# Routing and scatter moved into the delta rule of a one-core delta-rule and mixture-of-experts kernel

## What is computed

```python
# delta rule, k_n = k / (|k| + 1e-6), per batch and head
for t in range(S):
    y[t] = q[t] @ state
    state = state + beta[t] * outer(k_n[t], v[t] - k_n[t] @ state)
# experts: x is y as (3072, 384)
logits = x @ w_gate
e_idx = argmax(logits); gate_w = softmax(logits)[e_idx]
eom = 1 / (1 + exp(-(x @ w_output_gate)))
out[t] = gate_w * eom[t, e] * (relu(x[t] @ w1[e]) @ w2[e])      # e = e_idx[t]
# last layer
return maximum(maximum(out @ m1, out @ m2), out @ m3) @ w_out
```

## Time and profile before

| | before |
|---|---|
| runs, us | 1153.38, 1154.95, 1155.44 |
| median, us | 1154.95 |
| the profiled execution, us | 1154.56 |
| its span, us | 1152.8 |
| busy: PE, PEld, DVE, ACT, POOL, us | 1012.1, 887.3, 482.1, 366.7, 324.4 |
| mean granted clock of TensorE | 0.963 |
| stores of expert blocks (y_sorted<-y_sb) | 28 |
| memory read and written | 61.82 MB, 22.81 MB |

### The profile page before, as it was taken

The page is one execution under the profiler, slowest core; times in us unless marked ns, Lnnn a source line. Parts: engine busy times, 40 slices in busy tenths (PEclk is TensorE's granted clock), DMA queues, the critical chain, the costliest instruction groups (busy, mean ns, idle before and its releaser), DMA issues. The chain is left out here.

```text
span 1152.8 us, 30762 instructions
## 1 busy us (share of the span) xinstructions
PE 1012.1 (88%) x13236; PEld 887.3 (77%) x13236; DVE 482.1 (42%) x922; ACT 366.7 (32%) x731; POOL 324.4 (28%) x226
## 2 busy tenths in 40 slices
PE   1789999999998999810899999999599999999999
PEld 1678878888887888710799999999578888888888
DVE  3455555555555554360344344344242314242321
ACT  0255545555554555410222222222121212122211
POOL 2232333233422421046545255453420101000000
PEclk9999999999999999955899999999889999999999
DMA  8712121220212100016324344432211000100000
GB/s 267 269 54 63 28 60 40 62 63 26 63 40 62 41 20 19 2 42 232 136 81 155 122 151 151 150 124 82 89 49 35 28 34 20 34 20 28 10 19 28
DMA packets 59394, 86.37 MB, mean 75 GB/s; under 512 B 29200, under 2 KB 54288, under 8 KB 56720
## 3 DMA queue, kind: packets, MB, share of 16 engines
q1 hardware_dynamic: 53616, 48.46, 13.1%
q0 software_dynamic: 5664, 36.18, 9.2%
HBM read 61.82 MB, written 22.81 MB: 73 GB/s over the span
## 5 line engine op out<-in xcount | busy, mean ns | idle before, releaser
L1029 PE MATMUL hb<-early,last_h 128*128 128x512 f32 x648 | 203.8, 396 | 4.7 <-ACT o_sb L1143 3.5
L1029 PEld LDWEIGHTS hb<-early,last_h 128*128 128x128 f32 x648 | 120.5, 189 | 30.8 <-ACT o_sb L1143 2.7
L1029 PE MATMUL hb<-early,last_l 128*128 128x512 f32 x324 | 126.9, 392 | 0.0
L480 DVE TENSOR_TENSOR p<-bank,cf 128x512 f16<-128x512 f32 x96 | 66.0, 688 | 45.1 <-PE bank L283 44.8
L283 PEld LDWEIGHTS bank<-t,n_hi 64*64 64x64 f16 x2688 | 66.2, 111 | 21.1 <-issue 5.7
L1167 DVE TENSOR_TENSOR m<-hb,m 128x512 f32<-128x512 f32 x36 | 24.9, 691 | 131.4 <-PE hb L1029 131.4
L283 PE MATMUL bank<-t,n_hi 64*64 64x64 f16 x2688 | 71.6, 195 | 4.6 <-issue 3.9
L1029 PE MATMUL ob<-wo_h,early 128*128 128x384 f32 x288 | 74.2, 335 | 0.0
L1029 PEld LDWEIGHTS hb<-early,last_l 128*128 128x128 f32 x324 | 61.3, 189 | 13.2
L951 POOL TENSOR_TENSOR late<-w_raw,late 128x3072 fp32r<-128x3072 f32 x8 | 54.4, 6801 | 56.3 <-DVE late L923 56.0
L585 POOL COPY x_all<-y_tile 128x384 f32<-128x384 f32 x24 | 12.1, 503 | 205.3 <-ACT y_tile L451 205.3
(11 more groups left out here) (155 smaller groups left out, 2191.4 us busy)
## 6 DMA issues: line engine op xcount, KB each, us to landing
w_raw<-w POOLq DMA_DIRECT2D x14, 1536.0 KB, 7.6
kq_t<-qh SPq DMA_DIRECT2D x24, 256.0 KB, 3.3
x_sorted<-zeros SPq DMA_DIRECT2D x32, 192.0 KB, 1.9
x_in<-x_sorted SPq DMA_DIRECT2D x29, 192.0 KB, 2.4
y_sorted<-y_sb SPq DMA_DIRECT2D x28, 192.0 KB, 1.9
k_raw<-kt_in SPq DMA_DIRECT2D x24, 192.0 KB, 3.5
k_own<-kh SPq DMA_DIRECT2D x24, 192.0 KB, 3.3
v_in<-vh SPq DMA_DIRECT2D x24, 192.0 KB, 3.3
```

The lines of the kernel that those rows point to most:

```text
L480: dve.tensor_tensor(p16[st][:], pb, mask_of(lv), ALU.mult).then_inc(prod_out[st], 1)
L1029: ins = pe.matmul(out, a[x], b[y], start=first and i == 0, stop=last and i == 2, skip_group_check=True)
```

## The change

**Choice, rank and scatter of each tile move into the walk.** `CHAIN` gets three parts behind "lg": "rank" one slot later, "slot" two slots later and "send" five slots later. In "lg" VectorE now also takes the tile's maximum, marks and breaks ties, and writes `chosen` (four more operations). In "rank" TensorE multiplies a triangular matrix with `chosen` and ones with `counted`, the counts of all tiles so far, 8 columns each, in a free corner of the bank. In "slot" VectorE picks the row number and adds the tile to `counted` (four operations). In "send" GpSimd scatters the tile from `y_tile`, which is now double, instead of copying it to `x_all`. "ks" of the next step waits until "place" of "slot" has read the bank (`routed`), and the copy into `y_tile` waits for the scatter of two steps before. Since the counts are not known yet, each expert has an area of 26 blocks in `x_sorted`, and the slot is a place in it; SyncE adds the shift of the area (`off`) when it loads a block.

```diff
-    CHAIN = {0: ("ks", 0), 2: ("z", 0), 4: ("up", 0), 6: ("ks", 1), 8: ("z", 1), 10: ("up", 1), 12: ("yt", 0), 14: ("lg", 0)}
-    NORM = {1: [0], 2: [1], 3: [2], 5: [3], 6: [4], 7: [5], 8: [6], 9: [7, 8], 10: [9]}
+    CHAIN = {0: ("ks", 0), 2: ("z", 0), 4: ("up", 0), 6: ("ks", 1), 8: ("z", 1), 10: ("up", 1), 12: ("yt", 0), 14: ("lg", 0),
+             15: ("rank", 0), 16: ("slot", 0), 19: ("send", 0)}
+    NORM = {1: [0], 2: [1], 3: [2], 4: [10], 5: [3], 6: [4], 7: [5], 8: [6], 9: [7, 8], 10: [9], 12: [11], 13: [13], 14: [12]}
...
-                for of, off in ((a, 0), (c, SLOTS), (b, 2 * SLOTS)):
+                for of, off in ((b, 2 * SLOTS), (c, SLOTS), (a, 0)):
...
-                    pe.wait_ge(logit_out[st], k)
+                    pe.wait_ge(routed[st], 5 * k - 1)
...
+            elif what == "rank":
+                pe.wait_ge(chosen_ready[st], k + 1)
+                if 2 * k + st >= 1:
+                    pe.wait_ge(counted_ready, 2 * k + st)
+                pe.sem_inc(passed_pe, 1)
+                pe.matmul(out[:, X + P - E:X + P], tri16, chosen[:, 2 * k + st, :], start=True, stop=False, skip_group_check=True)
+                pe.matmul(out[:, X + P - E:X + P], ones16, counted[:], start=False, stop=True,
+                          skip_group_check=True).then_inc(rank_done[st], 1)
...
+            elif what == "slot":
+                to = 2 * k + st
+                dve.wait_ge(rank_done[st], k + 1)
+                dve.tensor_tensor(place[st][:], yb[st][:, X + P - E:X + P], chosen[:, to, :], ALU.mult).then_inc(routed[st], 1)
...
-            if what == "yt":
-                pool.wait_ge(y_out[st], 2 * k + 2)
-                pool.tensor_copy(x_all[:, 2 * k + st, :], y_tile[st][:]).then_inc(x_out[st], 1)
+            if what == "send":
+                to = 2 * k + st
+                pool.wait_ge(slot_ready[st], k + 1)
+                if k >= 1:
+                    pool.wait_ge(rows_sent[st], 16 * k)
+                pool.indirect_dma_start(xs, bass.IndirectOffsetOnAxis(ap=rows_at[:, to:to + 1], axis=0),
+                                        y_tile[par][st][:], None).then_inc(rows_sent[st], 16)
```

```diff
-        with sp.Fori(0, MAXB + 1) as g:
-            sp.dma_start(xs[bass.ds(P * g, P), :], zeros[:]).then_inc(xs_zeroed, 16)
-
-        with sp.Fori(TILES, MAXB + 1) as g:
-            sp.dma_start(ys[bass.ds(P * g, P), :], zeros[:]).then_inc(xs_zeroed, 16)
...
+        sp.wait_ge(zeroed, 16 * BLANK)
+        sp.wait_ge(tabled, 8)
+        row = sp.value_load(table[0:1, 2, 0:1], min_val=0, max_val=N)
+        sp.dma_start(xs[bass.ds(row, MINB * P), :].rearrange("(n p) x -> p n x", p=P),
+                     zeros[:].unsqueeze(1).broadcast_to((P, MINB, X))).then_inc(zeroed, 16)
+        sp.wait_ge(zeroed, 16 * BLANK + 16)
...
+        begin = 1
+        for e in range(E):
+            if e + 1 < E:
+                row = sp.value_load(table[0:1, 2, e + 1:e + 2], min_val=P * AREA * (e + 1), max_val=P * AREA * (e + 1) + N)
+                sp.dma_start(xs[bass.ds(row, MINB * P), :].rearrange("(n p) x -> p n x", p=P),
+                             zeros[:].unsqueeze(1).broadcast_to((P, MINB, X))).then_inc(zeroed, 16)
+            off = sp.value_load(table[0:1, 0, e:e + 1], min_val=0, max_val=AREA * e)
```

```diff
-            load_qv(k, k % 2)
+            for st in range(2):
+                if k + 1 < STEPS:
+                    load_own(k + 1, (k + 1) % 2, st)
+                load_qv(k, k % 2, st)
```

```diff
-                if t >= 2:
-                    pe.wait_ge(o_out, NT * n + t - 1)
+                pe.wait_ge(o_out, NT * n + t + 1)
...
-            pe.wait_ge(o_out, NT * n + NT)
```

431 lines of the change are left out of this document (234 added, 197 removed).

## The result

The changed kernel takes 1135.33 us (median of 4 runs, 1133.08 to 1137.52), the kernel before 1154.16 (1150.75 to 1155.44): a ratio of 0.9841 [0.9811, 0.9871], 18.8 us less. I had forecast 1110, with 1102 to 1121 as the range. The profiled run took 1136.08 us, with a span of 1134.3; the span before was 1152.8.

| stage | before, us | after, us | difference | forecast |
|---|---|---|---|---|
| start to the end of the last logits product | 493.7 | 515.6 | +21.8 | +3.2 |
| gap to the first xt_bank | 56.1 | 11.1 | -45.0 | -44.4 |
| experts, to the first ob | 281.0 | 282.2 | +1.2 | 0 |
| last layer, first ob to the end | 321.9 | 325.4 | +3.5 | -3.5 |

What follows compares the result with a forecast made beforehand. TensorE's queue was taken to bound the delta rule and experts, with a 56.1 us gap between. 0 + 2 + 1.2 - 44.4 + 0 - 3.5 = -44.7 from 1154.56 gave 1109.9, called 1110 us; range 1102 to 1121.

Steps and rivals of the forecast that it cites:

- Start: First loads, ahead of every engine's first work: fewer zeroing DMAs and a smaller wr change nothing, 0 us, between -1 and +1.
- Steady delta rule: Delta rule's steps: added TensorE products and VectorE operations mostly hidden, +2 us, between -6 and +10.
- rival 1: Delta rule: VectorE's routing operations push masks into TensorE's way, +10 us instead of +2, 1118 to 1120 us; chance 0.14.
- GpSimd, 0: Delta rule: GpSimd's 24 scatters replace 24 copies and are hidden, 0 us; without cover up to 5.9 us a step.
- the rule against the change: Skill's rule that GpSimd and VectorE contend for SBUF: scatters beside split pieces would be long ones; no size added.
- Tail: Delta rule's last step: stream 1's ks waits behind stream 0's rank, +1.2 us, between 0 and +3.
- Gap: Between last logits product and experts: 56.1 us shrinks to 11.7 (bounds 9.5 and 17), -44.4 us.
- Experts: Expert stage: no tile added to the 28, gates and table reads covered, 0 us; without cover +7.
- Last layer: Last layer: TensorE no longer waits for the copy of the last output, -3.5 us, between -3.5 and 0.
- rival 2: Delta rule: scatter and VectorE hold each other, 2 us per scatter, +48 us, 1158 us, slower than before; chance 0.03.
- Rival 3: Start of experts: after a shorter rest TensorE's clock keeps its higher level, -3.5 us and another 2, 1104 us; chance 0.11.
- rival 4: Gap stays 20 us or more, or borders between experts pay 7 us: 1118 to 1125 us; chance 0.10.

Runs made afterwards that it cites:

- a3: Changed kernel with expert 1's weight reload and VectorE's splits of expert 0's weights both moved behind the walk: 1150.02 us, ratio to before 0.9923.
- a2: Changed kernel with only the two reloads of expert 1's weights moved behind the walk, out of the tenth step: 1139.41 us, ratio to before 0.9848.
- d4: Changed kernel with buffers at the addresses of the kernel before, plus 32 short TensorE products ahead of the walk: 1116.08 us, ratio to before 0.9653.
- e1: Changed kernel with buffers placed as before, 32 short TensorE products ahead of the walk, and y_sorted's zero stores at the start: 1115.27 us, ratio 0.9646.
- c2: Changed kernel with each scatter issued twice, the second into a tensor nothing reads: 1147.92 us, ratio to before 0.9933.
- a4: Changed kernel with SyncE's 14 zero stores to y_sorted all at the start, ahead of the expert weights' loads: 1135.34 us, ratio to before 0.9811.
- b4: Changed kernel with SyncE's loads in the old order, both streams' keys ahead of q and v: 1136.67 us, ratio to before 0.9820.
- b1: Changed kernel unaltered, run and profiled again: 1138.82 us, ratio to before 0.9821.
- b2: Changed kernel with expert and last-layer buffers at their SBUF addresses in the kernel before, the delta rule's a multiple of 4096 bytes off: 1127.21 us, ratio 0.9756.
- b3: Changed kernel with each of VectorE's routing operations in the delta rule issued a second time into scratch: 1141.57 us, ratio to before 0.9857.
- e2: Changed kernel with buffers placed as in the kernel before, plus 96 short TensorE products ahead of the walk: 1131.34 us, ratio to before 0.9761.

## Why the prediction failed, step by step

**Start, 0: right.** The root from which the nine steps are counted came 0.6 us earlier (67.2 us instead of 67.8).

**Steady delta rule, +2: the step that failed.** It was +17.7 us over the nine steps: stalls for instructions 17.5 - 12.7 = +4.8; TensorE's wait for "chosen" +2.1; the clock 0.40 x 23.9 = +9.6; fixed work the remaining +1.2. The counted parts (two products per stream and step, VectorE's eight operations, splits, scatters) came to +3.3 against the +2 forecast. Of these, +2.1 is the wait for "chosen", and it comes from the split pieces, which I had put "in slots where VectorE still has some idling": in front of the logits copy it has none (a3). The chain behind the logits is otherwise covered in these steps, as forecast. I had even the outer bound, +10, from VectorE's operations (rival 1), and that was not it. What I left out stood in the page as "issue". These were 12.7 us of the nine steps before, and I took them for a constant, and the clock with them. The rival that said the clock would change looked only at the gap.

**Was it the routing, then?** The two profiles of after have 17.5 and 20.4 us of stalls, the two of before 12.7 and 13.3. In the changed kernel as it stands the reload in the tenth step goes with some 7 us (a2), but the same reload costs nothing there in d4 and e1. So what a stall costs, and whether the clock falls behind it, is mostly where the fetches fall: with nothing else moved the sum goes from 13.2 to 20.8 us. The kernel before has its share of this luck too: its second profile has 6.8 us of half clock where the first has none. Why most placements of the new program have more stalls than the old one is open; scatters (c2), zero stores (a4) and load order (b4) each do not explain it.

**GpSimd, 0, and the rule against the change: right on the path, wrong in size.** VectorE's split pieces were mis-sized: 0.55 us forecast for a subtraction, 0.68 to 1.82 measured. VectorE's timeline, then GpSimd's beside it:

```profile
198.88 0.60 DVE L578 TENSOR_TENSOR counted<-counted,chosen 128x8 f16<-128x8 f16 x1
...
208.56 1.81 DVE L638 TENSOR_TENSOR early<-w_raw,early 128x512 fp32r<-128x512 f32 x1
212.84 0.68 DVE L638 TENSOR_TENSOR early<-w_raw,early 128x512 fp32r<-128x512 f32 x1
```
```profile
198.64 0.83 POOL L685 TENSOR_TENSOR kn<-k_raw,nrm 128x384 f32<-128x384 f32 x1 [13.08 <-DVE nrm L606]
...
208.36 1.46 POOL L718 TENSOR_TENSOR ksq<-k_raw 128x768 f32<-128x768 f32 x1
209.78 1.27 POOL L700 TENSOR_TENSOR n_kb_a<-k_own,beta_k 128x384 f32<-128x384 f32 x1
```

Beside GpSimd's operations the same subtraction takes 1.81 us instead of 0.68, and an addition of 8 columns 0.60 instead of the 0.15 that it takes alone; it ends with GpSimd's kn. The Trainium skill, "GPSIMD Engine Reference", section 8 Key points, says that GpSimd contends with VectorE instructions that have two SBUF inputs, and both of these have: here the trace agrees, where for casts beside scatters I had found nothing to pay. These long ones are off the path: the subtraction that TensorE waits behind is the other, of 0.68 us (a3). No split piece ran beside a scatter, and no scatter behind the first took over 1.1 us, so that the rule's long scatters were not put to the test.

**Tail, +1.2: mechanism right, size short.** Stream 1's ks started 0.20 us behind the other stream's logits, now 1.74: +1.5 against +1.3. But from the last root to the last logits' end it was 100.1 us instead of 95.3, +4.8, with stalls of 1.01 and 0.78 us at 481 and 495 us, and the last 8.9 us, not 5.0, at 1.2 GHz.

**Gap, -44.4: right.** -45.0.

**Experts, 0: right in what it names,** no tile more and no wait for x_in. The +1.2 us is within what one program does from run to run: b1, the same kernel, has 281.3 us, +0.3.

**Last layer, -3.5: the wait is gone and worth 4.9 us** (b2), but the new buffers displaced the operands, +8.4. I read the diff for instructions and not for what its buffers do to the addresses of others.

**The rivals.** Rival 1 named the right stage and 1118 to 1120 us, by a cause that did not act: TensorE waits for VectorE's masks as long as before (3.8 and 3.2 us), and in the nine steps without the splits for nothing of the routing (a3). The scatter's rival 2 did not come: 1.0 us on GpSimd, hidden. Rival 3 looked at the clock behind the gap: 27.3 us at half clock instead of 68.3, but the experts began with 7.3 us of it where they had begun with 7.2, so nothing was gained; rival 4's gap did not come.

## What to carry to other kernels

Where TensorE is busy for 94% of a stage, sum its "issue" idle and look at the instruction queue before calling a change hidden: new loads beside dense short products can delay the next piece of instructions, the stalls can take the clock with them, and a few dozen dummy products in an idle place move the pieces at no cost (d4), for better or worse (e2). To ask whether a chain of operations is on the path, take something away or make the chain itself longer: copies that wait for nothing slip between its links (b3). A gain in the gap and a loss in the stage before it are two results; report them apart. After any change of buffers compare the start addresses of the operands of products that the change does not touch, and put small new buffers where they displace nothing.
